# A fetch block per expert body on TensorE, and a weight split of VectorE in two halves

## The reference, cut to what matters

```python
def _moe_ref(x, w_in, w_out):
    h = x @ w_in                                  # 1536 x 512 @ 512 x 2048
    g = h * (1.0 / (1.0 + np.exp(-1.702 * h)))
    return (g @ w_out)

def _moe2_ref(x, w_gate, w1, w2, capacity):
    logits = x @ w_gate
    expert_idx = np.argmax(logits, axis=1)
    ...
    h = np.maximum(np.einsum('ecd,edf->ecf', disp, w1), 0.0)   # 8 experts, 512 x 1024
    y = np.einsum('ecf,efd->ecd', h, w2)                        # 1024 x 512
    ...
            out[i] = gate_w[i] * y[expert_idx[i], pos[i]]
```

## Time and profile before

| | us |
|---|---|
| timed runs, median of 3 | 534.48 |
| lowest and highest | 533.99, 534.58 |
| profiled execution, own time | 539.34 |
| its span, first to last instruction | 537.6 |
| TensorE busy in the span | 512.2 (95%) |
| VectorE busy | 291.8 (54%) |
| ScalarE busy | 239.4 (45%) |
| mean granted TensorE clock | 0.985 |

### The profile page before, as it was taken

How to read it: one execution, slowest core, us unless ns; L and a number is a source line. 1 busy time by engine, 2 the same in 40 slices (tenths; PEclk the granted TensorE clock), 3 DMA queues, 4 the chain that set the end, 5 groups by cost and what they waited for, 6 DMA issues and landing times.

```text
span 537.6 us, 8647 instructions
## 1 busy us (share of the span) xinstructions
PE 512.2 (95%) x3159; PEld 433.5 (81%) x3159; DVE 291.8 (54%) x563; ACT 239.4 (45%) x424; POOL 185.5 (34%) x210
## 2 busy tenths in 40 slices
PE   8899889999999999999999999999998898999993
PEld 8898678888888878888887878897877788898882
DVE  6798554445333343223555554755466878647751
ACT  3797644343232222123443433423355757756620
POOL 2787300000000003000000460063245999998842
PEclk9899999999999999999999999999998999899997
DMA  8689699500000002001222443224693997875100
GB/s 282 193 257 280 227 336 321 167 0 1 1 0 1 2 0 80 1 0 40 78 79 80 156 123 111 81 80 140 222 342 115 336 337 243 280 279 212 45 26 32
DMA packets 28299, 75.07 MB, mean 140 GB/s; under 512 B 5455, under 2 KB 5455, under 8 KB 28240
## 3 DMA queue, kind: packets, MB, share of 16 engines
q1 hardware_dynamic: 23808, 67.63, 38.5%
q0 software_dynamic: 4000, 6.32, 3.2%
q10 hardware_dynamic: 432, 0.34, 0.2%
HBM read 61.12 MB, written 19.96 MB: 151 GB/s over the span
## 4 chain that ended last, share of the span: by engine, by line
PE 89%; issue 4%; DVE 3%; ACT 1%; DMA 1%; POOL 1%; SPq 0%; POOLq 0%; ACTq 0%
PE bank L1280 9%; PE bank L1282 9%; PE bank L1281 9%; PE bank L1324 8%; PE bank L1325 8%; PE bank L1326 8%; PE bank L1293 7%; PE bank L1245 3%; PE bank L1568 3%; PE bank L1570 3%; PE bank L1569 3%; PE bank L1566 3%; PE bank L1295 3%; PE bank L1272 2%; PE bank L1435 2%
## 5 line engine op out<-in xcount | busy, mean ns | idle before, releaser
L541 POOL DMA_INDIRECT dispatched_rows<-rows,slot_idx x12 | 14.1, 1172 | 273.1 <-issue 149.9
L368 POOL TENSOR_TENSOR w_lo<-raw,w_hi 128x256 fp32r<-128x256 f32 x100 | 88.9, 923 | 16.7 <-ACT w_hi L352 16.7
L901 DVE SCALAR_TENSOR_TENSOR g<-g,bank 128x512 f32<-128x512 f32 x48 | 33.0, 687 | 108.8 <-ACT g L632 106.7
L632 ACT ACTIVATE g<-bank 128x512 f32<-128x512 f32 x48 | 28.6, 597 | 135.3 <-PE bank L1282 135.3
L352 ACT ACTIVATE w_hi<-raw 128x1024 fp32r<-128x1024 f32 x80 | 82.8, 1052 | 0.0
L368 DVE TENSOR_TENSOR w_lo<-raw,w_hi 128x1024 fp32r<-128x1024 f32 x55 | 72.8, 1323 | 9.7 <-ACT w_hi L352 9.5
L1280 PE MATMUL bank<-x_hi,w_hi 128*128 128x512 f32 x192 | 77.0, 401 | 0.9 <-DVE w_lo L368 0.9
L1324 PE MATMUL bank<-w_hi,g_hi 128*128 128x512 f32 x192 | 76.0, 396 | 1.5 <-issue 1.5
L1325 PE MATMUL bank<-w_lo,g_hi 128*128 128x512 f32 x192 | 75.8, 395 | 0.0
L1326 PE MATMUL bank<-w_hi,g_lo 128*128 128x512 f32 x192 | 75.8, 395 | 0.0
L1282 PE MATMUL bank<-x_hi,w_lo 128*128 128x512 f32 x192 | 75.6, 394 | 0.0
(11 more groups left out here) (153 smaller groups left out, 899.6 us busy)
## 6 DMA issues: line engine op xcount, KB each, us to landing
raw<-expert_units SPq DMA_DIRECT2D x64, 512.0 KB, 5.7
raw<-dense_units SPq DMA_DIRECT2D x16, 512.0 KB, 7.5
dispatched_rows<-empty SPq DMA_DIRECT2D x26, 257.0 KB, 11.7
slot_rows<-dispatched_rows SPq DMA_DIRECT2D x26, 257.0 KB
tile_in<-attention_tiles SPq DMA_DIRECT2D x12, 384.0 KB, 4.7
tile_in<-attention_tiles SPq DMA_DIRECT2D x12, 336.0 KB, 5.3
queries<-attention_tiles SPq DMA_DIRECT2D x12, 256.0 KB, 4.7
mask<-masks ACTq DMA_DIRECT2D x1, 288.0 KB, 4.1
```

What stands on the lines that cost most here:

```text
L368: last = engine.tensor_tensor(w_lo[u % RING][:, part], raw[u % RING][:, part], w_hi[u % RING][:, part].bitcast(F32), ALU.subtract)
L901: dve.scalar_tensor_tensor(g32[i % 2][:, :], g32[i % 2][:, :], 1.0, h_bank[i % 2][:, :], ALU.add, ALU.mult).then_inc(s_g, 1)
```

## The change

Two things are changed. Every body of an expert now starts at slot 0 of a 256-slot block (`offset=0`), and the table `BODY_AT` is gone. And VectorE's `split_lo` behind f = 2 becomes two, one for the first 512 columns of the unit behind f = 2, one for the other 512 behind f = 4 (`LOW_STEPS`); its semaphore is raised after the second.

```diff
-    LOW_STEP = 2
+    LOW_STEPS = (2, 4)
...
-    BODY_AT = {P: 0, P + HALF: 120, 2 * P: 80, 2 * P + HALF: 64, 3 * P: 48}
...
-        def split_lo(engine, u):
+        def split_lo(engine, u, parts=1, some=None):
             engine.wait_ge(s_whi, u + 1)
-            parts = POOL_PARTS if by_pool(u) else 1
-            for n in range(parts):
+            for n in range(parts) if some is None else some:
                 part = slice(n * UC // parts, (n + 1) * UC // parts)
                 last = engine.tensor_tensor(w_lo[u % RING][:, part], raw[u % RING][:, part],
                                             w_hi[u % RING][:, part].bitcast(F32), ALU.subtract)
-            last.then_inc(low_done(u)[0], 1)
+            if some is None or parts - 1 in some:
+                last.then_inc(low_done(u)[0], 1)
...
-                    if e and f == LOW_STEP:
+                    if e and f in LOW_STEPS:
                         for u in splits_of(e)[:1]:
-                            split_lo(dve, u)
+                            split_lo(dve, u, len(LOW_STEPS), (LOW_STEPS.index(f),))
...
                 with nc.body(name + "pad"):
-                    pe.addr_align(PE_FETCH, offset=BODY_AT[wide], max_nops=0)
+                    pe.addr_align(PE_FETCH, offset=0, max_nops=0)
                     pe.br(label)
```

More of the change, by code:

```diff
@@ L564, in _ @@
                 if by_pool(u):
-                    split_lo(pool, u)
+                    split_lo(pool, u, POOL_PARTS)
             zeros(NBLK - 1)
@@ L1591, in announce, with leave @@
                 return announced
-            def leave(jump, count, w, name, behind):
-                if behind is None:
+            def leave(jump, count, w, name, label):
+                if label is None:
                     return jump()
-                label, wide = behind
                 pe.br_cond(count > w, name + "pad", name + "jump")
@@ L1608, in laid_behind @@
                 if at_ < len(WIDTHS) * E:
-                    e, w = at_ // len(WIDTHS), WIDTHS[at_ % len(WIDTHS)]
-                    return f"expert{e}_{w}", w
+                    return f"expert{at_ // len(WIDTHS)}_{WIDTHS[at_ % len(WIDTHS)]}"
             def go_on(e, announced, name, behind):
@@ L1670, in _ @@
             count.append(load_count(pe, 7))
-            go_on(0, announced, "first", (f"expert0_{WIDTHS[0]}", WIDTHS[0]))
+            go_on(0, announced, "first", f"expert0_{WIDTHS[0]}")
             for e in range(E):
```

## The result

The change makes the kernel slower. The median of six timed runs is 543.35 us, against 535.34 us for the kernel before, timed beside it; the ratio of the runs is 1.0142 with a 95% interval of 1.0116 to 1.0168, so 7.6 us (6.2 to 9.0). The profiled execution after has a span of 542.6 us; that of before had 537.6.

What follows compares the result with a forecast made beforehand. TensorE, busy for 95% of the span, was taken to bound the kernel. The halves gain 4.4 us, bodies at slot 0 lose 9.0, so 4.6 us slower: 534.48 + 4.6 = 539.1 us, range 529.5 to 545.

Steps and rivals of the forecast that it cites:

- the half clock: Behind the new gaps at the jumps out of experts 3 and 6, TensorE's clock halves: 1.6 us each, 3.2 us lost.
- loss for expert 6: Late jump out of expert 6 delays expert 7's first matmul: 1.9 us lost, bounds 1.4 to 2.9.
- The halves: VectorE's split in halves shortens TensorE's waits for gx_lo and ends expert 4's half clock: 4.4 us gained, bounds 1.6 to 5.5.
- The crossing rule: A hinted code block is asked for only when the sequencer enters the block holding the jump, usable 3.5 us later.
- The gap of expert 1: Jump out of expert 1 done at 404.2 in place of 403.75: 0.7 us lost, up to 1.4 with the weights' DMA.
- The gap of expert 3: Jump out of expert 3 done at 444.3, now 441.6: 2.7 us without cover, 3.2 us lost with DMA traffic.
- part two: Bodies moved to slot 0 make the jumps out of width 192 late: 9.0 us lost, bounds 6.2 to 12.2.
- the late fetch of expert 1: At expert 1's jump, 3.9 us perhaps only in the profiled run; if so, the slot-0 loss costs up to 3.9 more.
- A: Rival: the code fetch isn't tied to the crossing, so slots change nothing; 4.4 us faster, 530.1 us; chance 0.13.
- B: Rival: bodies starting on a block boundary get their target early, expert 1's gap and half clock go; 526.2 us; chance 0.09.
- C: Rival: expert 5's later crossing meets weight traffic and its fetch waits too; 8.2 us slower, 542.7 us; chance 0.07.

Runs made afterwards that it cites:

- one_block: The change with both ladders shortened so a width-192 body and its jumps to widths up to 256 lie in one block; 533.29 us against 537.25 before.
- no_hint: The change without any prefetch hint and without the ladders that carry them; 561.76 us against 537.25 for the kernel before, ratio 1.0462.
- slot_184: The kernel before with bodies of width 192 at slot 184 in place of 120; ratio 0.9933 against before.
- slot_40: The kernel before with bodies of width 192 at slot 40 in place of 120; ratio 1.0058 against before.
- layout_only: The change with VectorE's subtraction whole, every body at slot 0; 547.08 us against 536.54 for the kernel before, ratio 1.0175.
- split_only: The change's split in halves with the slots of the kernel before; 532.89 us against 536.54 for the kernel before, ratio 0.9930.
- slot_224: The kernel before with bodies of width 192 at slot 224 in place of 120; ratio 1.0077 against before.

## Why the prediction was right and wrong

The direction, the slots as the cause and the places of the stalls held; the size was too small, 4.6 us forecast and 7.6 (6.2 to 9.0) measured. The measured median of 543.35 us lies 4.2 above the forecast 539.1; 0.9 of that is the kernel before itself, at 535.34 beside it and not at 534.48. The step of the prediction that failed is the half clock, a stretch of 1.6 us behind every gap over 1.42 us; a term of 0.8 us was missing, and an over-large loss for expert 6 and too small a gain for the halves hid part of it.

- **The crossing rule**: right. Forecast: jumps out of experts 3 and 6 of about 3 us, and a fetch behind the exit ladder. Measured 4.22 and 2.91 us, the fetches behind the jumps' start. The runs with four other slots, one_block and no_hint each could have overturned it, and didn't. What it gave as the reason for the delay held only in part: the hinted block was to queue behind the weights' DMA, and with that traffic nearly gone 4.8 to 8.1 us of 7.4 to 11.4 were left. From the crossing to the end of the jump the change took 4.4, 4.7 and 3.0 us in experts 1, 3 and 6, where the sum had 3.5 and a share for traffic.
- **The gap of expert 1**: 0.7 more forecast, 1.47 measured, just past the bound of 1.4. Jump and fetch: 3.98 us, the fetch began 1.6 us behind the jump, with the last weights still coming.
- **The gap of expert 3**: 3.2 forecast, 3.96 measured (bounds 2.7 to 4.5). **Expert 6**: 1.9 forecast, 1.39 measured.
- **The half clock**: the step that failed, twice. I priced every stretch at 1.6 us, from those of before. Behind the gaps of 3.75 and 3.96 us they were 6.1 and 5.2 us long and cost 3.05 and 2.6 us; I had counted expert 1's as "there already". Before, the clock was still at full when the matmuls began again behind the gap of 2.28 us (the first took 0.47 us); in the change it had fallen within the gap (the first took 0.77 us), as the stage 402:404, without a matmul, shows by its granted clock of 0.88:

```profile
402.00:404.00 2.00, 0.00 (x0) 0.88 0.04 8
```

  And I set a rule, a gap over 1.42 us brings one, which put one behind expert 6 as well. There was none behind its gap of 1.39. Forecast 3.2 us for the new ones, less 1.7 for expert 4's; measured 2.35 net against the 1.5 forecast. The net is that near by luck: the two long stretches cost 2.4 us more than their price, and the one that didn't come saved 1.6.
- **The halves**: the waits of the five hidden blocks fell by 3.5 us, where 2.7 were forecast, and expert 4's half clock went, as said. A half took 747 ns in the mean, not the 692 of the row that I took, and a whole one 1287 after, so the second half pays some 200 ns more and not 60. Alone, the split gained 3.8 us (2.4 to 5.2) for the forecast 4.4.
- **Not in the sum**: 0.8 us more waiting at the starts of the bodies that follow width 128. The prediction says that three kinds of waits are left, 7.2 us together; the same view has two more of 0.8 us each (line 1568 for gx_lo, line 1532 for issue), so this term was put at nothing without a reason. Why it grows to a third wait is read from the half clock in expert 5's start before; no run isolates it.
- **From the profile to the median**: I carried a difference of 4.6 us over from one profiled execution. The trace pair shows 6.6 us in the experts and 1.6 us less ahead of them, and with the layout alone 9.4 us (7.2 to 11.5) were measured for a forecast of 9.0. So the sum for part two was near in total, though its terms were off both ways.
- Whether before's timed runs have the late fetch of expert 1, as the prediction asked, stays open in part. slot_184, whose profiled execution doesn't have that stall, gained 3.6 us (2.4 to 4.8), about the 3.9 of the stall with its half clock, which speaks for it. But the mean granted clock was 0.985 in the profiled execution of before, and 0.991 in the median of the 28 executions of before beside slot_184, so most of those had less of the half clock.
- **Rivals.** A (nothing depends on the slot) and B (the target comes early) fell with the result. B's idea is right for a body that really lies in one block: one_block shows it. C (expert 5's fetch late as well) did not come: its jump took 0.41 us after.

## What to carry to other kernels

In this kernel a branch hint is served only once the sequencer has entered the code block that holds the hinted jump, and often not at once, so look at which block the jump is in, not the body. The crossing 11 us ahead of the jump was at times too late, most of all in expert 1; 15 us ahead it was late in none of the three profiled executions with slot 184. Nor should it come before the following block is there (with the crossing 32 slots behind the start, the sequencer got past it 3.4 to 5.5 us behind the start). Nine slots of exit ladder over the border cost what no hint at all costs. In the profile such a stall has no semaphore: it is a wait for "issue", a branch of microseconds in the sequencer's rows, and a packet on the instruction queue right behind it. And where one engine's long step stands in a chain that is nearly as tight as the bound, halve it and put the parts where the chain has slack; it gained 0.7% here.

## What the runs showed of the hardware

- A hinted block is fetched 1.8 to 6.9 us behind the start of a body that lies in one block (before and one_block). In one of two blocks the fetch comes behind the crossing, by 7.4 to 11.4 us in experts 1, 3 and 6 with slots 120 and 184, by 4.8 to 8.1 with the weights' traffic nearly gone, and by at most 1.3 us once (slot_40, expert 6). The part that isn't traffic has no explanation here.
- A jump whose block is asked for only on the exit ladder or by itself takes 2.9 to 6.7 us; the jump with its block there costs 0.30 to 0.42 us. A jump that has to wait is done 2.3 to 2.7 us after its packet starts; what varies is how long the packet takes to start: 0.6 to 4.3 us behind the jump's start in the change, layout_only and no_hint.
- The granted clock doesn't follow the length of the gap alone. It fell to 0.50 behind gaps of 1.42 us (before), 3.32 us (slot_40), 3.75 and 3.96 us (the change), but stayed at 1.00 behind gaps of 1.69 us (split_only), 1.76 us (slot_40) and 2.84 us (slot_224). The last two, with the stage behind each:

```profile
443.97 0.47 PE L1568 MATMUL bank<-w_hi,gx_hi 128*128 128x512 f32 x1 [1.76 <-issue]
...
444.00:449.00 5.00, 5.00 (x24) 1.00 0.03 3
```

```profile
423.30:428.00 4.70, 4.70 (x24) 1.00 0.16 47
```

The rule of 1.42 us that the prediction drew from two stretches was no rule.
